# Attention with a fused mixture and MLP on one core: the last head's output is turned and its row sums are made directly in front of a head's first values

## The chip, the cores and the metric

The kernel runs on one core of a Trainium2 chip. The time is the device time of one execution in microseconds (us), and lower is better. Five engines work side by side, each through its own queue in program order, and meet only through semaphores. TensorE (PE) multiplies, VectorE (DVE) and ScalarE (ACT) work on what it leaves in PSUM, GpSimd (POOL) works on tiles in SBUF, and SyncE (SP) issues the transfers.

## The reference, cut to what matters

Three stages follow each other. The change lies in the first; the second and third (a mixture of four causal attention experts, and a two-layer MLP) take its output.

```
batch, n_heads, seq, head_dim = (4, 8, 1152, 64)
q_pool = q.reshape(B, H, S // 2, 2, D).mean(axis=3)         # 576 queries of 1152
scores = scale * np.matmul(q_pool, k.transpose(0, 1, 3, 2)) # 576 x 1152 for each of 32 heads
scores = scores - np.max(scores, axis=-1, keepdims=True)
attn = np.exp(scores)
attn = attn / (np.sum(attn, axis=-1, keepdims=True) + 1e-09)
x = np.matmul(attn, v)
```

Everything is float32. There are 32 heads (4 batches of 8), numbered 0 to 31 here.

## The kernel before

`attention` walks through the 32 heads in a hand-written software pipeline. While head h makes its exponentials, head h + 1 gets its maxima.

The **maxima** (`max_piece`, L329 to L341 on PE, L597 to L601 on DVE) are 15 pieces a head, numbered 0 to 14: PE writes a 128 x 384 block of scores into one of two PSUM banks (L339), and DVE reduces it to one number a row (L600). The two banks alternate. Piece n therefore waits at L338 until DVE has reduced piece n - 2 (`max_freed`), and DVE's reduction of n waits for PE's piece n.

The **scores** of a key tile j (`score(h, j)`, L343 to L361, nine a head) are two matmuls of L349 and two of L358 into one of two double banks. ACT makes the exponentials from them (L529, `exp_done`). `score(h, j)` waits for the exponentials of tile j - 2.

The **values** (`values`, L363 to L376) multiply the exponentials by v into `o_bank`, first for key tiles 0 to 3 (`EARLY` = 4), later for tiles 4 to 8. Each wants a tile's `exp_done`.

After a head, ACT copies the output out of `o_bank` as `oT` (L537, `o_copied`), and DVE adds up the probabilities over the keys (`add_late` and `sum_blocks`, L609 to L628), for which it waits for POOL's additions (`add_tiles`, L239 to L252). The result lies in `group_sums`. One head later PE makes `turn_out` (three fp32 transposes of `oT`, L383) and `sum_rows` (one fp32 matmul of `group_sums`, L388, which the trace counts as two), both into the bank `turn`. When `sum_rows` is done, DVE's `normalise` (L630 to L655) takes the reciprocal and writes the head's rows to `x_all`. DVE has it in its queue between the reductions of pieces 8 and 9 (L679). The next keys may be turned into `turn` only when `normalise` has set `x_ready` (`claim_turn`, L289).

Order on PE is the order of the loop at L403. Before the change `turn_out` stands between pieces 5 and 6, `sum_rows` between pieces 6 and 7, and `score(h, 4)` between 7 and 8; then come `values(h, range(EARLY))` and pieces 9 and 10. Head 0 has no earlier head, so its loop runs without the two.

In head 31 there are no more maxima. In their place stands the beginning of the experts (`first(0, ...)`): `x` 0 to 3 and `x_last` transpose `x_all` (L1225), ACT and DVE split the result (L39, L44). Their banks are two in turn: `x` 3 takes the bank of `x` 1, and `x_last` that of `x` 2, when DVE's split of it is done.

In heads 8 to 14 POOL also splits the experts' weights after its additions (`split_expert`, `split_values`, `split_V`, L274 to L279).

Of the kernel before, what the change touches and what calls it, by code (L numbers as in the profile page):

```python
# [53 lines left out]
def attention(nc, q, k, v, x_all, x_ready, ident, ident_r, ready, ahead):  # L54
# [42 lines left out]
    def max_no(h, n):  # L97
        return h * MAX_USES + n

    ctx = ExitStack()  # L100
    with ctx:
# [186 lines left out]
        def _(pe):  # L288
# [54 lines left out]
            def score(h, j):  # L343
                u, n = h % 2, h * KT + j
                if n >= 2:
                    pe.wait_ge(exp_done, n - 1)
                out = scores[n % 2]
                for half in range(2):
                    nc.tensor.matmul(out[:, half, 0:HALF], kT[u][:, j * P:(j + 1) * P],  # L349
                                     qT[h % 3][:, half * HALF:(half + 1) * HALF],  # L350
                                     start=True, stop=False)
                if j == 0:
                    pe.wait_ge(k1_copied, h + 1)
                    for use in (Q_LO, Q_LO_LAST):
                        at = max_no(h, use)
                        pe.wait_ge(max_freed[at % 2], at // 2 + 1)
                for half in range(2):
                    mm = nc.tensor.matmul(out[:, half, 0:HALF], kT1[u][:, j * P:(j + 1) * P],  # L358
                                          qTm[u][:, half * HALF:(half + 1) * HALF],
                                          start=False, stop=True)  # L360
                mm.then_inc(scores_ready, 1)  # L361

            def values(h, tiles):  # L363
                u = h % 2
                if tiles[0] == 0:
                    pe.wait_ge(v_loaded[u], 16 * (h // 2 + 1))
                    pe.wait_ge(qa_copied, min(h + 3, HEADS))
                for j in tiles:
                    pe.wait_ge(exp_done, h * KT + j + 1)
                    for half in range(2):  # L370
                        at = half * SHIFT
                        mm = nc.tensor.matmul(o_bank[half * D:(half + 1) * D, at:at + HALF],  # L372
                                              v_raw[u][:, j, :],
                                              pT[:, j, half * HALF:(half + 1) * HALF],
                                              start=(j == 0), stop=(j == KT - 1))
                    mm.then_inc(pv_done, 1)  # L376

            def turn_out(h):

                pe.wait_ge(o_copied, h + 1)  # L380
                claim_turn(("out", h))
                for t in range(3):
                    nc.tensor.transpose(turn[:, t * P:(t + 1) * P], oT[:, t * P:(t + 1) * P],  # L383
                                        ident[:, :])

            def sum_rows(h):
                pe.wait_ge(groups_summed, h + 1)
                mm = nc.tensor.matmul(turn[:, 3 * P:3 * P + QT * GROUPS], all_groups[:, :],  # L388
                                      group_sums[:, :], start=True, stop=True)
                mm.then_inc(turned, 1)  # L390
# [12 lines left out]
            for h in range(HEADS - 1):  # L403
                more2 = h + 2 < HEADS

                def maxima(a, z):
                    for at in range(a, z):
                        max_piece(h + 1, at)

                score(h, 0)  # L410
                maxima(0, 2)
                turn_keys(h + 1, "kc", [KT - 1])
                score(h, 1)
                maxima(2, 3)
                score(h, 2)
                maxima(3, 4)
                if more2:
                    turn_queries(h + 2)
                maxima(4, 5)
                score(h, 3)  # L420
                maxima(5, 6)
                if h > 0:
                    turn_out(h - 1)
                maxima(6, 7)
                if h > 0:
                    sum_rows(h - 1)
                maxima(7, 8)
                score(h, 4)
                maxima(8, 9)
                values(h, range(EARLY))  # L430
                maxima(9, 11)
                score(h, 5)
                maxima(11, 12)
                if more2:
                    turn_keys(h + 2, "ka", range(0, 4))
                maxima(12, 13)
                score(h, 6)
                maxima(13, 14)
                score(h, 7)
                maxima(14, 15)  # L440
                score(h, 8)
                if more2:
                    turn_keys(h + 2, "kb", range(4, 8))
                turn_q_lo_m(h + 1)
                values(h, range(EARLY, KT))

            first, h = ahead.tensor(pe, first=True), HEADS - 1
# [4 lines left out]
            first(0, ("x", 1))  # L452
            score(h, 3)
            first(0, ("x", 2))
            turn_out(h - 1)
            sum_rows(h - 1)
            first(0, ("x", 3))
            score(h, 4)
            first(0, ("x_last",))
            values(h, range(EARLY))  # L460
            score(h, 5)
            first(0, ("qk", 0, 0))
# [133 lines left out]
        def _(dve):  # L596
# [33 lines left out]
            def normalise(h):  # L630
                dve.wait_ge(turned, turn_no["out", h] + 1)
                sums = turn[:, 3 * P:3 * P + QT * GROUPS].rearrange("p (t g) -> p t g", g=GROUPS)
                nc.vector.tensor_tensor(picked[:, :, :], sums, own_group[:, :].unsqueeze(1
                                        ).to_broadcast([P, QT, GROUPS]), ALU.mult
                                        ).then_inc(sums_picked, 1)
                dve.wait_ge(sums_picked, 2 * h + 1)
                nc.vector.tensor_reduce(sum_inv[:, :], picked[:, :, :], AX.X, ALU.add
                                        ).then_inc(sums_picked, 1)
                dve.wait_ge(sums_picked, 2 * h + 2)
                nc.vector.reciprocal(sum_inv[:, :], sum_inv[:, :]).then_inc(inverted, 1)  # L640
                dve.wait_ge(inverted, h + 1)
                cols = slice(h * D, (h + 1) * D)
                src = turn[:, 0:3 * P].rearrange("p (t a d) -> p a t d", a=2, d=D)
                by = sum_inv[:, 0:QT - 1].rearrange("p (a t) -> p a t", a=2)
                nc.vector.tensor_tensor(
                    x_all[:, 0:QT - 1, cols].rearrange("p (a t) d -> p a t d", a=2),
                    src[:, :, 0:2, :], by.unsqueeze(3).to_broadcast([P, 2, 2, D]), ALU.mult
                    ).then_inc(x_full, 1)
                nc.vector.tensor_tensor(x_all[0:LAST, QT - 1, cols], src[0:LAST, 1, 2, :],
                                        sum_inv[0:LAST, QT - 1:QT].to_broadcast([LAST, D]),  # L650
                                        ALU.mult)
                dve.wait_ge(x_full, h + 1)
                nc.vector.tensor_tensor(x_all[0:SHIFT, 2, cols], src[0:SHIFT, 0, 2, :],
                                        sum_inv[0:SHIFT, 2:3].to_broadcast([SHIFT, D]),
                                        ALU.mult).then_inc(x_ready, 1)  # L655
# [29 lines left out]
            def add_tile(j, n):  # L685

                total, h = p_sum[:, 0:SQ], HEADS - 1
                dve.wait_ge(exp_done, h * KT + j + 1 if j < KT else HEADS * KT)
                if j == KT:
                    dve.wait_ge(part_summed, h * (len(ON_POOL) - 1) + len(LAST_ON_POOL) - 1)  # L690
                if n == 0:
                    ins = nc.vector.scalar_tensor_tensor(
                        total, pT[:, LAST_ON_POOL.stop, :], EPS / P, pT[:, j, :], ALU.add, ALU.add)
                else:
                    dve.wait_ge(p_summed, h * SUM_STEPS + n)
                    ins = nc.vector.tensor_tensor(total, total, pT[:, j, :], ALU.add)
                ins.then_inc(p_summed, 1)

            first, h = ahead.vector(dve, first=True), HEADS - 1
            first(0, ("x", 0))  # L700
            first(0, ("x", 1))
            first(0, ("x", 2))
            normalise(h - 1)
            first(0, ("x", 3))
            first(0, ("x_last",))
            add_tile(5, 0)
            first(0, ("qk", 0, 0))
            add_tile(6, 1)
# [1121 lines left out]
```

## Time and profile before

| | us |
|---|---|
| median of 3 runs | 1202.93 (1200.16 to 1203.36) |
| the profiled execution, its own time | 1200.94 |
| its span, first to last instruction | 1199.2 |
| PE, DVE, ACT, POOL busy | 1141.5, 650.0, 543.9, 521.9 |
| attention: turning of the first head's output to that of the last | 45.1 to 533.4 |

Times in the trace are microseconds from the start of the span. The ends of matmuls are modelled: a matmul begins before the one ahead of it has ended, so the distance from start to start tells what PE spends on it. A row of the timeline merges instructions of one kind ("x4"); the bracket gives the idle time ahead and what ended it. Where PE waits for a bank, this shows at the weight load (PEld) or at the matmul, as idle time with DVE as its releaser, and often only as a larger distance from start to start.

### The profile page before, as it was taken

The numbers are of one execution on the slowest core, as the hardware profiler recorded it, in microseconds if no ns is written. First come the engines' busy times: TensorE is split into PE (matmuls) and PEld (weight loads), VectorE is DVE, ScalarE is ACT, GpSimd is POOL, SyncE is SP. The second block draws the span as 40 slices with busy tenths as digits, with TensorE's granted clock in tenths as the row PEclk, the third lists the DMA queues.
The fourth block names the chain that finished last, engine by engine and source line by source line (L and its number), as shares of the span: only waits on it lengthen the run. The fifth ranks groups of instructions, "written<-read, shape, count | busy, mean of one in ns | idle before, by whom it ended". The sixth has DMA issues, their size and how long they took to land. (4 is left out here: it accounts for less than half of the span.)

```text
span 1199.2 us, 19574 instructions
## 1 busy us (share of the span) xinstructions
PE 1141.5 (95%) x7232; PEld 956.5 (80%) x7232; DVE 650.0 (54%) x1380; ACT 543.9 (45%) x1131; POOL 521.9 (44%) x560
## 2 busy tenths in 40 slices
PE   6999999989999999998899999789999999999998
PEld 4777777777778777777777777579898989899896
DVE  4788877767888888856556565554121212122120
ACT  4666665565666666546565656633020201111010
POOL 5788899998888888734333333200000000000000
PEclk9999999999999999998999999989999999999999
DMA  8111112211122111003001010132100101010000
GB/s 203 50 54 51 57 60 60 60 43 49 60 60 61 60 60 40 21 1 141 1 1 41 1 41 27 41 123 84 53 1 15 39 1 52 0 52 0 27 1 27
DMA packets 47559, 54.56 MB, mean 46 GB/s; under 512 B 10992, under 2 KB 29424, under 8 KB 46960
## 3 DMA queue, kind: packets, MB, share of 16 engines
q1 hardware_dynamic: 47472, 53.42, 14.3%
q8 instruction: 53, 0.87, 0.3%
q14 instruction: 34, 0.28, 0.1%
HBM read 43.97 MB, written 9.44 MB: 45 GB/s over the span
## 5 line engine op out<-in xcount | busy, mean ns | idle before, releaser
L600 DVE TENSOR_REDUCE part_max<-psA 128x1 f32<-128x384 f32 x480 | 258.4, 556 | 67.9 <-PE psA L339 46.8
L529 ACT ACTIVATE pT<-psA 128x576 f32<-128x576 f32 x288 | 187.7, 652 | 165.5 <-PE psA L358 156.4
L251 POOL TENSOR_TENSOR pT<-pT 128x576 f32<-128x576 f32 x157 | 225.0, 1433 | 25.8 <-ACT pT L529 4.0
L339 PE MATMUL psA<-kT,qT 128*128 128x384 f32 x480 | 174.5, 388 | 11.3 <-DVE part_max L600 10.9
L372 PE MATMUL psA<-pT,v_raw 128*64 128x288 f32 x1152 | 153.9, 412 | 0.0
L1706 ACT ACTIVATE hid_hi<-psC 128x384 fp32r<-128x384 f32 x96 | 47.2, 492 | 198.4 <-PE psC L1631 198.3
L349 PE MATMUL psA<-qT,kT 128*128 128x288 f32 x576 | 133.5, 314 | 0.0
L1725 DVE SCALAR_TENSOR_TENSOR hid_lo<-psC,hid_hi 128x384 fp32r<-128x384 f32 x96 | 53.5, 558 | 137.8 <-ACT hid_hi L1706 137.8
L358 PE MATMUL psA<-qTm,kT 128*128 128x288 f32 x576 | 124.1, 297 | 0.2 <-ACT qTm L515 0.2
L339 PEld LDWEIGHTS psA<-kT,qT 128*128 128x128 f32 x480 | 88.4, 193 | 40.0 <-DVE part_max L600 21.2
L372 PEld LDWEIGHTS psA<-pT,v_raw 128*64 128x64 f32 x1152 | 77.1, 137 | 53.1 <-issue 6.4
L349 PEld LDWEIGHTS psA<-qT,kT 128*128 128x128 f32 x576 | 99.2, 190 | 18.3 <-issue 14.0
L1647 PE MATMUL psC<-w_hi,hid_hi 128*128 128x512 f32 x288 | 113.7, 395 | 0.0
L1647 PE MATMUL psC<-w_hi,hid_lo 128*128 128x512 f32 x288 | 112.5, 391 | 0.0
L1647 PE MATMUL psC<-w_lo,hid_hi 128*128 128x512 f32 x288 | 112.3, 390 | 0.0
L358 PEld LDWEIGHTS psA<-qTm,kT 128*128 128x128 f32 x576 | 93.4, 191 | 0.5 <-issue 0.5
L1631 PE MATMUL psC<-uT_hi,w_hi 128*128 128x384 f32 x384 | 83.1, 339 | 1.4 <-DVE uT_lo L44 1.4
L1631 PE MATMUL psC<-uT_lo,w_hi 128*128 128x384 f32 x384 | 82.9, 338 | 0.0
L1631 PE MATMUL psC<-uT_hi,w_lo 128*128 128x384 f32 x384 | 82.3, 337 | 0.0
L1088 POOL TENSOR_SCALAR moe_probs<-moe_probs,moe_sum_inv,gate 128x128 f32<-128x128 f32 (+4 forms) x80 | 53.3, 666 | 65.3 <-DVE moe_sum_inv L1461 61.2
L1351 ACT ACTIVATE moe_probs<-psB,moe_neg_max 128x128 f32<-128x128 f32 (+4 forms) x80 | 45.5, 569 | 68.0 <-DVE moe_neg_max L1474 67.3
L1631 PEld LDWEIGHTS psC<-uT_hi,w_hi 128*128 128x128 f32 x384 | 68.6, 190 | 2.2 <-DVE uT_lo L44 1.8
(162 smaller groups left out, 1931.7 us busy)
## 6 DMA issues: line engine op xcount, KB each, us to landing
k_raw<-in_k SPq DMA_DIRECT2D x32, 288.0 KB, 2.9
v_raw<-in_v SPq DMA_DIRECT2D x32, 288.0 KB, 2.8
q_raw<-in_q SPq DMA_DIRECT2D x32, 256.0 KB, 3.2
w_raw<-in_moe_w_ch SPq DMA_DIRECT2D x1, 4096.0 KB, 14.0
u_rows<-x_all SPq DMA_DIRECT2D x16, 256.0 KB, 2.0
w_raw<-in_moe_w_ch SPq DMA_DIRECT2D x16, 256.0 KB, 2.7
u_first<-u_rows SPq DMA_DIRECT2D x3, 768.0 KB, 4.5
u_second<-u_rows SPq DMA_DIRECT2D x3, 768.0 KB, 4.8
```

What stands on the lines that cost most here:

```text
L251: nc.gpsimd.tensor_tensor(pT[:, KT, :], pT[:, KT, :], pT[:, j, :], ALU.add).then_inc(part_summed, 1)
L339: nc.tensor.matmul(maxes[n % 2][:, 0:PIECE], qT[h % 3][:, t * P:(t + 1) * P], kT[u][:, c * PIECE:(c + 1) * PIECE], start=True, stop=True). ...
L349: nc.tensor.matmul(out[:, half, 0:HALF], kT[u][:, j * P:(j + 1) * P], qT[h % 3][:, half * HALF:(half + 1) * HALF], start=True, stop=False)
L358: mm = nc.tensor.matmul(out[:, half, 0:HALF], kT1[u][:, j * P:(j + 1) * P], qTm[u][:, half * HALF:(half + 1) * HALF], start=False, stop=True)
L372: mm = nc.tensor.matmul(o_bank[half * D:(half + 1) * D, at:at + HALF], v_raw[u][:, j, :], pT[:, j, half * HALF:(half + 1) * HALF], start=( ...
L529: nc.scalar.activation(pT[:, j, :].rearrange("p (a c) -> p a c", a=2), scores[n % 2][:, :, 0:HALF], ACT.Exp, scale=0.5 * float(D) ** -0.5) ...
L600: nc.vector.tensor_reduce(part_max[u][:, t, c:c + 1], maxes[n % 2][:, 0:PIECE], AX.X, ALU.max).then_inc(max_freed[n % 2], 1)
L1088: nc.gpsimd.tensor_scalar(p, p, sum_inv[0:rows, e, i:i + 1], gate[b % 2][0:rows, i, e:e + 1], ALU.mult, ALU.mult).then_inc(scaled, 1)
L1631: mm = nc.tensor.matmul(up[f % 4], w1_s[w][:, k, f * P:(f + 1) * P], uT[x][:, k, :], start=((w, x, k) == (*PARTS3[0], 0)), stop=((w, x, k) ...
L1647: mm = nc.tensor.matmul(down[t], hid[h][:, f, t * P:(t + 1) * P], w2_s[w][:, f, :], start=(n == 0), stop=(n == 3 * FC - 1))
L1706: nc.scalar.activation(hid[0][:, f, :], up[f % 4], ACT.Relu).then_inc(up_hi, 1)
L1725: nc.vector.scalar_tensor_tensor(hid[1][:, f, :], up[f % 4], 0.0, hid[0][:, f, :].bitcast(F32), ALU.max, ALU.subtract).then_inc(up_lo, 1)
```

## The change

`turn_out(h - 1)` and `sum_rows(h - 1)` move behind piece 8, to stand directly in front of `values(h, range(EARLY))`. `score(h, 4)` moves from behind piece 7 to behind piece 6. In head 31 the two stand behind `x_last` instead of behind `x` 2, and DVE's `normalise` of head 30 moves behind the splits of `x` 3 and `x_last`. No instruction is added or taken away, and DVE's order in the other heads is as it was.

```diff
@@ -418,15 +418,13 @@
                     turn_queries(h + 2)
                 maxima(4, 5)
                 score(h, 3)
-                maxima(5, 6)
+                maxima(5, 7)
+                score(h, 4)
+                maxima(7, 9)
+
                 if h > 0:
                     turn_out(h - 1)
-                maxima(6, 7)
-                if h > 0:
                     sum_rows(h - 1)
-                maxima(7, 8)
-                score(h, 4)
-                maxima(8, 9)
                 values(h, range(EARLY))
                 maxima(9, 11)
                 score(h, 5)
@@ -452,11 +450,11 @@
             first(0, ("x", 1))
             score(h, 3)
             first(0, ("x", 2))
-            turn_out(h - 1)
-            sum_rows(h - 1)
             first(0, ("x", 3))
             score(h, 4)
             first(0, ("x_last",))
+            turn_out(h - 1)
+            sum_rows(h - 1)
             values(h, range(EARLY))
             score(h, 5)
             first(0, ("qk", 0, 0))
@@ -700,9 +698,9 @@
             first(0, ("x", 0))
             first(0, ("x", 1))
             first(0, ("x", 2))
-            normalise(h - 1)
             first(0, ("x", 3))
             first(0, ("x_last",))
+            normalise(h - 1)
             add_tile(5, 0)
             first(0, ("qk", 0, 0))
             add_tile(6, 1)
```

PE's queue in the loop of head 1 before the change, from score 3 to the pieces behind the values. `kT0,qT2` are the operands of the maxima's pieces (of head 2), `qT1,kT1` and `qTm1,kT11` those of the scores (of head 1); L383 is `turn_out`, L388 `sum_rows`, L372 the values:

```order
L349 MATMUL psA<-qT1,kT1 128x288 x2
L358 MATMUL psA<-qTm1,kT11 128x288 x2
L339 MATMUL psA<-kT0,qT2 128x384
L383 MATMUL psA<-ident,oT 128x128 x3
L339 MATMUL psA<-kT0,qT2 128x384
L388 MATMUL psA<-group_sums,all_groups 128x20
L339 MATMUL psA<-kT0,qT2 128x384
L349 MATMUL psA<-qT1,kT1 128x288 x2
L358 MATMUL psA<-qTm1,kT11 128x288 x2
L339 MATMUL psA<-kT0,qT2 128x384
L372 MATMUL psA<-pT,v_raw1 64x288 x8
L339 MATMUL psA<-kT0,qT2 128x384 x2
```

Each of the four pieces 5 to 8 (L339) has other work of PE in front of it. The same place after the change:

```order
L349 MATMUL psA<-qT1,kT1 128x288 x2
L358 MATMUL psA<-qTm1,kT11 128x288 x2
L339 MATMUL psA<-kT0,qT2 128x384 x2
L349 MATMUL psA<-qT1,kT1 128x288 x2
L358 MATMUL psA<-qTm1,kT11 128x288 x2
L339 MATMUL psA<-kT0,qT2 128x384 x2
L383 MATMUL psA<-ident,oT 128x128 x3
L388 MATMUL psA<-group_sums,all_groups 128x20
L372 MATMUL psA<-pT,v_raw1 64x288 x8
L339 MATMUL psA<-kT0,qT2 128x384 x2
```

Pieces 6 and 8 now follow directly on pieces 5 and 7, score 4 alone stands between the two pairs, and L383 and L388 come between piece 8 and the values. This place recurs in heads 1 to 30; head 0 has it without L383 and L388.

PE's queue in head 31 before the change, from score 2 to the first values. L1225 are the transposes `x` 1, 2, 3 and, with 64 columns, `x_last`:

```order
L349 MATMUL psA<-qT1,kT1 128x288 x2
L358 MATMUL psA<-qTm1,kT11 128x288 x2
L1225 MATMUL psB<-ident,x_all 128x128 x4
L349 MATMUL psA<-qT1,kT1 128x288 x2
L358 MATMUL psA<-qTm1,kT11 128x288 x2
L1225 MATMUL psB<-ident,x_all 128x128 x4
L383 MATMUL psA<-ident,oT 128x128 x3
L388 MATMUL psA<-group_sums,all_groups 128x20
L1225 MATMUL psB<-ident,x_all 128x128 x4
L349 MATMUL psA<-qT1,kT1 128x288 x2
L358 MATMUL psA<-qTm1,kT11 128x288 x2
L1225 MATMUL psB<-ident,x_all 128x64 x4
L372 MATMUL psA<-pT,v_raw1 64x288 x8
```

And after the change, where the lines behind the loop have moved up by two (L1223 is L1225 of before):

```order
L349 MATMUL psA<-qT1,kT1 128x288 x2
L358 MATMUL psA<-qTm1,kT11 128x288 x2
L1223 MATMUL psB<-ident,x_all 128x128 x4
L349 MATMUL psA<-qT1,kT1 128x288 x2
L358 MATMUL psA<-qTm1,kT11 128x288 x2
L1223 MATMUL psB<-ident,x_all 128x128 x8
L349 MATMUL psA<-qT1,kT1 128x288 x2
L358 MATMUL psA<-qTm1,kT11 128x288 x2
L1223 MATMUL psB<-ident,x_all 128x64 x4
L383 MATMUL psA<-ident,oT 128x128 x3
L388 MATMUL psA<-group_sums,all_groups 128x20
L372 MATMUL psA<-pT,v_raw1 64x288 x8
```

The eight transposes of `x` 2 and `x` 3 now stand together, and L383 and L388 stand between `x_last` and the values.

## Rows read from the trace of the kernel before

**Rows 1.** The page: busy us of each engine, share of the span, instructions.

```profile
PE 1141.5 (95%) x7232; PEld 956.5 (80%) x7232; DVE 650.0 (54%) x1380; ACT 543.9 (45%) x1131; POOL 521.9 (44%) x560
```

**Rows 2.** One line's instructions, L388 on PE, stretches 168:288 and 287:503.

```profile
L388 PE MATMUL psA<-group_sums,all_groups x16: 181/224/267, 168.4 to 287.7; 128*128 128x20 f32 x16
...
L388 PE MATMUL psA<-group_sums,all_groups x30: 181/224/267, 287.7 to 502.1; 128*128 128x20 f32 x30
```

**Rows 3.** Timeline of PE in head 17: start, us, engine, line, operation.

```profile
302.35 0.34 PE L339 MATMUL psA<-kT,qT 128*128 128x384 f32 x1
302.53 0.49 PE L383 MATMUL psA<-ident,oT 128*128 128x128 f32 x3
...
303.03 0.29 PE L388 MATMUL psA<-group_sums,all_groups 128*128 128x20 f32 x2
303.34 0.44 PE L339 MATMUL psA<-kT,qT 128*128 128x384 f32 x1
...
304.14 0.34 PE L339 MATMUL psA<-kT,qT 128*128 128x384 f32 x1
304.41 2.16 PE L372 MATMUL psA<-pT,v_raw 128*64 128x288 f32 x16
306.50 0.62 PE L339 MATMUL psA<-kT,qT 128*128 128x384 f32 x2
```

**Rows 4.** Timeline of DVE in the same head, three windows.

```profile
302.73 1.06 DVE L600 TENSOR_REDUCE part_max<-psA 128x1 f32<-128x384 f32 x2 [0.15 <-PE psA L339]
...
304.52 0.56 DVE L600 TENSOR_REDUCE part_max<-psA 128x1 f32<-128x384 f32 x1
...
306.98 2.89 DVE L600 TENSOR_REDUCE part_max<-psA 128x1 f32<-128x384 f32 x5 [0.68 <-PE psA L339]
```

**Rows 5.** Timeline of head 0: PE, then PEld and DVE.

```profile
29.81 0.73 PE L339 MATMUL psA<-kT,qT 128*128 128x384 f32 x2
30.80 0.45 PE L339 MATMUL psA<-kT,qT 128*128 128x384 f32 x1 [0.26 <-DVE part_max L600]
31.08 0.43 PE L349 MATMUL psA<-qT,kT 128*128 128x288 f32 x2
...
31.62 0.33 PE L339 MATMUL psA<-kT,qT 128*128 128x384 f32 x1
...
30.09 0.19 PEld L339 LDWEIGHTS psA<-kT,qT 128*128 128x128 f32 x1 [0.23 <-DVE part_max L600]
...
30.19 1.02 DVE L600 TENSOR_REDUCE part_max<-psA 128x1 f32<-128x384 f32 x2
```

**Rows 6.** PE in head 0, the values.

```profile
31.88 2.16 PE L372 MATMUL psA<-pT,v_raw 128*64 128x288 f32 x16
```

**Rows 7.** Timeline of PE in head 31, then a row of DVE there.

```profile
516.70 0.49 PE L383 MATMUL psA<-ident,oT 128*128 128x128 f32 x3
517.03 0.30 PE L388 MATMUL psA<-group_sums,all_groups 128*128 128x20 f32 x2
517.24 0.66 PE L1225 MATMUL psB<-ident,x_all 128*128 128x128 f32 x4
...
518.37 0.45 PE L1225 MATMUL psB<-ident,x_all 64*128 64x64 f32 x4
518.74 2.16 PE L372 MATMUL psA<-pT,v_raw 128*64 128x288 f32 x16
...
516.49 0.69 DVE L44 TENSOR_TENSOR xT_lo<-psB,xT_hi 128x512 fp32r<-128x512 f32 x1 [0.34 <-ACT xT_hi L39]
```

**Rows 8.** PE behind the last `sum_rows`, of head 31.

```profile
535.07 0.30 PE L388 MATMUL psA<-group_sums,all_groups 128*128 128x20 f32 x2
535.21 0.31 PE L1235 MATMUL psB<-wvg_hi,xT_hi 128*64 128x260 f32 x1
```

**Rows 9.** POOL at the end of head 17.

```profile
313.32 1.42 POOL L218 TENSOR_TENSOR k_parts<-k_raw,k_parts 128x576 fp32r<-128x576 f32 x1 [1.61 <-ACT k_parts L483]
```

**Rows 10.** Waits in head 10's stretch, 184.7:201.3.

```profile
DVE p_sum L618 <- POOL pT L251: 1.3, 1, 1.3
```

## The prediction, on record before the changed kernel ran

> **What bounds the kernel now.** I read the page's busy line first: the reader is to see PE at 95% of the span, DVE at 54% and POOL at 44% [rows 1]. So what counts is the distance between starts on PE. Next came the spacing of `sum_rows` over the heads. In the stretch from 287.7 there are 15 of them (30 matmuls) with 214.4 us between the first and the last, 15.31 a head. In the stretch from 168.4 there are eight (16 matmuls) with 119.3 us between them, 17.04 a head, although PE does the same there [rows 2]. These seven periods are set by POOL: in head 10 the additions of `p_sum` on DVE wait 1.3 for POOL [rows 10], where in head 17 POOL itself has 1.61 idle [rows 9]. The others are PE's.
>
> Then the timelines of the place that changes, in heads 17 and 0. I count from the start of piece 5. In head 17 the values start at 304.41 - 302.35 = 2.06 [rows 3]. In head 0, which has neither `turn_out` nor `sum_rows`, they start at 31.88 - 29.81 = 2.07 [rows 5, 6]. This is the row that decides the case: the two operations cost nothing today. In head 0 PE stands idle instead, at piece 6 (0.23 ahead of its weight load) and at piece 7 (0.26 as the view counts it), both released by DVE [rows 5]. In head 17 piece 7 starts at 303.34, which is 0.05 behind the end of reduction 5 (302.73 + 0.56; the row of two, 1.06, ends at 303.79) [rows 3, 4]. So pieces 5 to 7 go at DVE's pace, and the transposes fill holes.
>
> **The change, part by part.** Nothing is added or taken away; the sum consists of holes that open and work that loses its cover. I build up heads 1 to 30 from piece 5, at 0.
>
> Piece 6 now follows at once. It needs reduction 4. Head 0 has this very sequence: 30.09 - 29.81 = 0.28 [rows 5]. Score 4 follows a piece that was just released: 31.08 - 30.80 = 0.28, and takes 31.62 - 31.08 = 0.54 [rows 5]. So piece 7 starts at 0.28 + 0.28 + 0.54 = 1.10. It needs reduction 5, which starts 0.38 behind piece 5 and ends at 0.94 [rows 3, 4]: no wait. That is the gain of the change: score 4 covers the wait at piece 7.
>
> Piece 8 follows at once too, and needs reduction 6. Reductions 5 and 6, back to back, take 1.02 [rows 5], so 6 ends at 0.38 + 1.02 = 1.40, and with the 0.05 of a release piece 8 starts at 1.45. PE could have had it at 1.10 + 0.18 (302.53 - 302.35) [rows 3] = 1.28: a new hole of 0.17, and another 0.10 because the work behind a released piece starts 0.28 and not 0.18 later.
>
> Now `turn_out` and `sum_rows` stand uncovered. `turn_out` starts at 1.45 + 0.28 = 1.73. From it to `sum_rows` PE takes 517.03 - 516.70 = 0.33 [rows 7]: 2.06. From `sum_rows` to the values: the trace has no such pair. The values start about 0.07 ahead of the modelled end of what precedes them, behind a piece (304.14 + 0.34 against 304.41) [rows 3] as behind `x_last` (518.37 + 0.45 against 518.74) [rows 7]. `sum_rows` lasts 0.29 or 0.30 [rows 3, 7], so I take 0.22. The values then start at 2.28, against 2.06: **0.22 us later a head**. From below: 0.14 to the next matmul, as behind the last `sum_rows` [rows 8], and 0.18 in place of 0.28 behind piece 8, which gives 2.10, or +0.04. From above: 0.31 behind `sum_rows`, as it is to piece 7 (303.34 - 303.03), and 1.06 for the two reductions [rows 3, 4], which gives 2.41, or +0.35.
>
> On the values' start the Trainium skill (TensorE: Matmul & The Clock Gate, Part 2, step 5, NX overlap) says that the drain of a matmul overlaps the fill of the next. By that the values should follow `sum_rows` at the 0.14 of the lower bound, and a head would lose 0.14. The trace disagrees at the values: both times they wait for nearly all of the modelled end. Step 1 of the same part of the Trainium skill's page says that PE pulls weight loads ahead of matmuls in flight; for a released piece the trace does not show it, since in head 0 the load of piece 6 begins at 30.09, on release. By that rule the 0.28 would be 0.18 and a head would lose 0.12.
>
> Is it given back later? DVE is not late: reduction 8 ends near 2.5 (it began at 2.17 before [rows 3, 4] and begins some 0.2 earlier), `turned` comes at 2.06 + 0.29 = 2.35, so `normalise` has no new wait, although it now depends on a matmul that stands directly ahead of it. After it DVE had 0.68 idle until reduction 9, which waits for piece 9 on PE [rows 4]; that only grows. Pieces 9 and 10 stand behind the values (306.50), and everything to the end of the head hangs on them. Score 4 is ready earlier, and so are its exponentials on ACT, but nobody waits for these. The keys' turning needs `x_ready`, which comes a little earlier. The exponentials behind score 5 come 0.22 later for POOL, which at the end of the head has 1.61 to spare [rows 9]. So PE keeps the 0.22.
>
> Where it counts: 30 heads have the new place, 7 of their periods are POOL's and swallow it (they lose 12 us to POOL, 119.3 - 7 x 15.31, much more than 7 x 0.22). 23 x 0.22 = **+5.1**.
>
> Head 0 has nothing to uncover: its piece 8 starts at 1.45, is released, so it lasts 0.44 to 0.45 (30.80's row) [rows 5], and the values follow 0.07 ahead of the end: 1.82 against 2.07, **-0.25**.
>
> Head 31: `turn_out` and `sum_rows` stood where `x` 3 would have waited for DVE anyway: it starts at 517.24, 0.06 behind DVE's split of `x` 1 (516.49 + 0.69) [rows 7]. That hole stays. The two now come between `x_last` and the values: 0.33 + 0.22, less about 0.09, since `turn_out` can start closer behind a transpose than the values do. **+0.46**, between 0.33 and 0.64. `normalise` behind two splits of DVE is hidden: the next addition waits for exponentials.
>
> The sum: 5.1 - 0.25 + 0.46 = +5.3. The profiled execution took 1200.94 (its span 1199.2 and 1.7 around it), so 1206.2. The median of the runs is 1202.93, 0.17% above it. On that scale the forecast is 1202.93 + 5.3 = **1208.2 us**. The bounds a head give 23 x 0.04 + 0.1 = +1.0 and 23 x 0.35 + 0.4 = +8.4: 1203.9 to 1211.3.
>
> **The rivals.**
> A dearer one: all 30 heads pay, because the delay comes behind the additions that POOL's chain needs. 30 x 0.22 + 0.2 = +6.8, 1209.7. Against it: POOL works through without waiting in these heads.
> A cheaper one: the released weight load or the change to the values costs less than I take. At 0.04 to 0.14 a head it is +1.1 to +3.4, say 1205.2, inside what a measurement can tell (0.3%, 3.6 us). For it: [rows 8]. Against it: both starts of the values.
> One on the other side, faster: PE's sum of work decides and not the pace of DVE. From `turn_out` to piece 7 the old order takes 303.34 - 302.53 = 0.81 [rows 3]; without piece 6 (0.18) that leaves 0.63 for two fp32 groups with fp32r matmuls on either side. Together in front of the fp32 values they take 0.33 + 0.14 = 0.47. That would save 0.16 in each of 23 heads, -3.7, so 1199.2. It decides if reductions 5 and 6 come early enough that piece 8 needs no wait, by 1.28 where I count 1.40. Against it: head 0's 2.07 without either group shows that the 0.63 was no cost.
> That the change does not do what it says can be left aside; the order of the queue shows it.
>
> **How the numbers follow.** My forecast 0.66, the dearer rival 0.12, the cheaper one 0.17, the faster one 0.05. Slower 0.78, same 0.17, faster 0.05. The range takes in both bounds of a head and a run's scatter (1200.16 to 1203.36 before): 1203.5 to 1211.5, which leaves out the faster rival and the tails.
>
> **What would show it.** In a middle head, from piece 5: piece 6 at 0.28, piece 7 near 1.10, piece 8 near 1.45 with DVE named as releaser, the values near 2.28; 15.53 a head in place of 15.31, and an unchanged 17.0 in the seven heads of POOL. Head 0's values at 1.82. Wrong would be: values at 2.06 or earlier (the sum of work decides), or 0.22 at the values and yet 15.31 a head (given back later, at DVE or POOL).

## The result and the profile after

The median went from 1200.96 to 1207.44 us in 15 runs of each. The ratio is 1.0047, with a 95% interval of 1.0035 to 1.0060: the change costs 4 to 7 us, about 5.6 (the two medians lie 6.5 apart). The forecast was +5.3. The profiled execution took 1209.26, its span is 1207.5. The granted clock of TensorE is 1.00, the upper of its two levels (2.4 GHz), up to the end of attention in the trace of before and in that of after, so it has no part in what attention loses.

The place that changed, in head 17 of the kernel after, is the counterpart of [rows 3] (start, us, engine, line, operation; L339 pieces, L349 the first two matmuls of score 4, L383 `turn_out`, L388 `sum_rows`, L372 values):

```profile
305.04 0.72 PE L339 MATMUL psA<-kT,qT 128*128 128x384 f32 x2
305.59 0.42 PE L349 MATMUL psA<-qT,kT 128*128 128x288 f32 x2
...
306.12 0.87 PE L339 MATMUL psA<-kT,qT 128*128 128x384 f32 x2
306.83 0.49 PE L383 MATMUL psA<-ident,oT 128*128 128x128 f32 x3
307.16 0.30 PE L388 MATMUL psA<-group_sums,all_groups 128*128 128x20 f32 x2
307.38 2.16 PE L372 MATMUL psA<-pT,v_raw 128*64 128x288 f32 x16
```

The values start 2.34 behind piece 5, where they started at 2.06. Next come the weight loads of the two pieces that follow directly on another (PEld), and DVE's reductions 5 and 6, 7 and 8, and the first step of `normalise`, counterparts of [rows 4]:

```profile
305.31 0.19 PEld L339 LDWEIGHTS psA<-kT,qT 128*128 128x128 f32 x1 [0.22 <-DVE part_max L598]
...
306.54 0.19 PEld L339 LDWEIGHTS psA<-kT,qT 128*128 128x128 f32 x1 [0.34 <-issue]
...
305.41 1.02 DVE L598 TENSOR_REDUCE part_max<-psA 128x1 f32<-128x384 f32 x2
...
306.50 1.09 DVE L598 TENSOR_REDUCE part_max<-psA 128x1 f32<-128x384 f32 x2
307.50 0.17 DVE L631 TENSOR_TENSOR picked<-psA,own_group 128x20 f32<-128x20 f32 x1
```

Piece 6 waits for reduction 4 (0.22 idle). Piece 8 waits for reduction 6, which ends at 305.41 + 1.02 = 306.43; its load begins at 306.54, with 0.34 idle ahead of it. The view puts that hole down to "issue" and names no engine. What ends in it is a wait that stands as an instruction of its own, of line 338 (`max_freed`), and that runs right behind the end of reduction 6:

```profile
L338 PEldq EVENT_SEMAPHORE  x1: 51/51/51, 306.5 to 306.5; - x1
```

`sum_rows` as it recurs, against [rows 2], for the heads of POOL and for those behind them:

```profile
L388 PE MATMUL psA<-group_sums,all_groups x16: 185/226/266, 173.1 to 291.6; 128*128 128x20 f32 x16
...
L388 PE MATMUL psA<-group_sums,all_groups x30: 185/226/266, 291.6 to 509.8; 128*128 128x20 f32 x30
```

Fourteen periods of 218.2 are 15.59 a head in place of 15.31. The seven periods of POOL take 118.5 in place of 119.3: they swallow the delay, although in most of these heads too the values start 2.35 behind piece 5. Head 31, the counterpart of [rows 7]:

```profile
522.77 0.66 PE L1223 MATMUL psB<-ident,x_all 128*128 128x128 f32 x4
523.81 0.66 PE L1223 MATMUL psB<-ident,x_all 128*128 128x128 f32 x4 [0.38 <-DVE xT_lo L44]
...
524.93 0.45 PE L1223 MATMUL psB<-ident,x_all 64*128 64x64 f32 x4
525.31 0.55 PE L383 MATMUL psA<-ident,oT 128*128 128x128 f32 x3
525.69 0.30 PE L388 MATMUL psA<-group_sums,all_groups 128*128 128x20 f32 x2
525.92 2.16 PE L372 MATMUL psA<-pT,v_raw 128*64 128x288 f32 x16
```

`x` 3 still starts 1.04 behind `x` 2, now with an open wait in between; before it was 517.24 [rows 7] - 516.20:

```profile
516.20 0.66 PE L1225 MATMUL psB<-ident,x_all 128*128 128x128 f32 x4
```

From `x_last` to the values it takes 0.99, where it took 0.37: +0.62.

The span grew by 8.3, more than the ratio of the runs. Of this, 1.2 is there before the changed place is reached for the first time (piece 5 of head 0's loop starts at 31.02 in place of 29.81), and 1.1 lies behind attention. Neither stands in the change, and both vary as much between kernels that do not differ there: over the twelve traces of this case piece 5 of head 0's loop starts between 28.4 and 31.2, and from head 31's first values to the end it takes 677 to 683 (680.5 before, 681.6 after), in the old order and the new one alike. The changed places themselves make up -0.2 (head 0), 22 x 0.275 = 6.1 (the periods of heads 1 to 8 and 16 to 29), and 0.9 from head 30 to the experts; the seven heads of POOL came out 0.8 shorter.

### The profile page after: what moved, and what is told of

Its sections match the earlier page's. It is cut to its first block and busy times, and to the rows that moved or that the text cites. A ratio compares the mean times of both kernels' runs of the same rounds, so it can differ in the third digit from the quotient of the medians.

```text
span 1207.5 us, 19574 instructions
## 1 busy us (share of the span) xinstructions
PE 1146.6 (95%) x7232; PEld 956.3 (79%) x7232; DVE 645.7 (53%) x1380; ACT 543.9 (45%) x1131; POOL 521.4 (43%) x560
## 5 line engine op out<-in xcount | busy, mean ns | idle before, releaser
L339 PE MATMUL psA<-kT,qT 128*128 128x384 f32 x480 | 172.4, 387 | 12.1 <-DVE part_max L598 8.7
L372 PE MATMUL psA<-pT,v_raw 128*64 128x288 f32 x1152 | 153.8, 412 | 0.0
L349 PE MATMUL psA<-qT,kT 128*128 128x288 f32 x576 | 133.4, 313 | 0.0
L339 PEld LDWEIGHTS psA<-kT,qT 128*128 128x128 f32 x480 | 88.2, 193 | 50.5 <-issue 25.4
L372 PEld LDWEIGHTS psA<-pT,v_raw 128*64 128x64 f32 x1152 | 77.0, 136 | 47.8 <-issue 0.2
L349 PEld LDWEIGHTS psA<-qT,kT 128*128 128x128 f32 x576 | 99.2, 190 | 18.3 <-issue 14.0
```

The source lines that it names most:

```text
L339: nc.tensor.matmul(maxes[n % 2][:, 0:PIECE], qT[h % 3][:, t * P:(t + 1) * P], kT[u][:, c * PIECE:(c + 1) * PIECE], start=True, stop=True). ...
```

## The experiments

Theory: **cover**. Without other work between the pieces PE waits for DVE at pieces 6 and 7, as head 0 of before shows. In the old order `turn_out` and `sum_rows` fill the wait at piece 6 and most of that at piece 7; the new order takes the fillers out, puts score 4 ahead of piece 7, and leaves waits open at pieces 6 and 8. Rivals: the **sum of work** on PE decides; or the **new neighbours** cost the 0.28 (fp32 transposes ahead of the values). Positions are read in head 17 from the start of piece 5, unless said otherwise. In heads 1 to 8 and 17 to 29 of a trace the start of the values agrees within 0.03, but for one head of one trace; "a head" is the mean period behind POOL's heads.

The first seven kernels were executed once each: 1207.85, 1212.93, 1210.05 and 1207.97 us for the two with added transposes, score 4 back, and the second wait moved, next to 1203.32 of before, then 1188.64, 1191.72 and 1204.28 (short reductions in the old and the new order, head 31 alone), next to a median of 1200.77 of before. One such time scatters by several us, more than most of these edits are worth, so the positions decide.

### Work added in the place of the transposes

```diff
-                for t in range(3):
+                for t in (0, 1, 2, 0, 1, 2):
                     nc.tensor.transpose(turn[:, t * P:(t + 1) * P], oT[:, t * P:(t + 1) * P],
```

In the old order: 

> The order of before, with turn_out's three transposes made twice (six transposes, the same result). One look, read in a middle head from the start of piece 5. Theory (cover: in the old order the transposes fill a wait of PE for DVE): the three extra transposes are 0.33 of PE's work, but about 0.15 to 0.2 of it fits into what is left of the wait ahead of piece 7, so the values start at 2.16 to 2.25 in place of 2.07, and a head lasts 15.4 to 15.5. Rival (sum of work: PE's own work decides, no cover): the full 0.33, values at 2.40, a head 15.65.

In the new order: 

> The order of after, with turn_out's three transposes made twice. Theory (cover: behind piece 8 nothing waits for DVE any more): the full 0.33 us, values at 2.68 in place of 2.35 behind the start of piece 5, 15.92 a head in place of 15.59. Rival (the 0.28 that the change costs is the price of new neighbours, and a wait is still there that takes up work): less than 0.33, values below 2.60.

The old order, with six transposes:

```profile
304.64 0.34 PE L339 MATMUL psA<-kT,qT 128*128 128x384 f32 x1
304.82 0.82 PE L383 MATMUL psA<-ident,oT 128*128 128x128 f32 x6
305.39 0.42 PE L339 MATMUL psA<-kT,qT 128*128 128x384 f32 x1
305.65 0.29 PE L388 MATMUL psA<-group_sums,all_groups 128*128 128x20 f32 x2
305.79 0.42 PE L339 MATMUL psA<-kT,qT 128*128 128x384 f32 x1
...
306.89 2.16 PE L372 MATMUL psA<-pT,v_raw 128*64 128x288 f32 x16
```

Values at 2.25, 15.50 a head: 0.33 of added work costs 0.19, the rest goes into what was left of the wait. Piece 7 now starts 0.14 behind `sum_rows` (305.79 - 305.65), where it stood 0.31 behind it in [rows 3]: 0.17 of wait was left there, and it is filled. The new order, with six:

```profile
308.42 0.72 PE L339 MATMUL psA<-kT,qT 128*128 128x384 f32 x2
...
311.09 0.46 PE L372 MATMUL psA<-pT,v_raw 128*64 128x288 f32 x2
```

Values at 2.67, 15.92 a head: the full 0.33. This is what the theory says, and it speaks against a wait being left behind piece 8.

### Score 4 back between pieces 7 and 8

```diff
-                maxima(5, 7)
+                maxima(5, 8)
                 score(h, 4)
-                maxima(7, 9)
+                maxima(8, 9)
```

> The order of after, with score 4 back between pieces 7 and 8 (pieces 5, 6, 7, score 4, piece 8, turn_out, sum_rows, values). It undoes the one part that is meant to help. Theory (cover): pieces as in head 0 of before, 6 at 0.29, 7 at 0.99, 8 at 1.81; turn_out 1.99, sum_rows 2.32, values 2.55, which is 0.48 later than before and 0.20 later than after; 15.79 a head. Rival (the place of score 4 does not matter, the price is only at the values): values at 2.35 as in after.

```profile
304.84 0.72 PE L339 MATMUL psA<-kT,qT 128*128 128x384 f32 x2
305.82 0.44 PE L339 MATMUL psA<-kT,qT 128*128 128x384 f32 x1 [0.26 <-DVE part_max L598]
...
306.63 0.34 PE L339 MATMUL psA<-kT,qT 128*128 128x384 f32 x1
306.81 0.49 PE L383 MATMUL psA<-ident,oT 128*128 128x128 f32 x3
307.13 0.30 PE L388 MATMUL psA<-group_sums,all_groups 128*128 128x20 f32 x2
307.36 2.16 PE L372 MATMUL psA<-pT,v_raw 128*64 128x288 f32 x16
```

The pieces stand as in head 0 of before [rows 5], with the same 0.26 for DVE, and the two operations come on top: values at 2.52, 15.76 a head. So moving them alone costs 0.46 a head, and the new place of score 4 gives back 0.17. The rival falls.

### DVE made faster

```diff
-                nc.vector.tensor_reduce(part_max[u][:, t, c:c + 1], maxes[n % 2][:, 0:PIECE],
+                nc.vector.tensor_reduce(part_max[u][:, t, c:c + 1], maxes[n % 2][:, 0:PIECE // 2],
```

In the old order: 

> The order of before, with DVE's reduction of each piece over 192 of its 384 columns (leaves half of the columns out of the maxima); PE's work is as before. A reduction should last about 0.36 in place of 0.56. Theory (cover: PE waits for DVE at piece 7): the wait goes, values at about 1.80 to 1.90 in place of 2.07 behind the start of piece 5. Rival (sum of work decides in the old order): 2.07 stays.

In the new order: 

> The order of after, with DVE's reduction of each piece over 192 of its 384 columns (leaves half of the columns out of the maxima). Theory (cover): without waits for DVE there is nothing to cover, so both orders cost the same work: values at 1.75 to 1.85, within 0.1 of the old order with the same short reductions, and a head as long or up to 0.15 shorter. Rival (the new neighbours cost the 0.28 by themselves): values 0.2 to 0.3 later than in the old order with short reductions.

Old order, then new order, from piece 5 to the values:

```profile
298.19 0.34 PE L339 MATMUL psA<-kT,qT 128*128 128x384 f32 x1
...
300.07 2.16 PE L372 MATMUL psA<-pT,v_raw 128*64 128x288 f32 x16
```

```profile
297.21 0.52 PE L339 MATMUL psA<-kT,qT 128*128 128x384 f32 x2
297.56 0.42 PE L349 MATMUL psA<-qT,kT 128*128 128x288 f32 x2
...
298.10 0.67 PE L339 MATMUL psA<-kT,qT 128*128 128x384 f32 x2
298.60 0.49 PE L383 MATMUL psA<-ident,oT 128*128 128x128 f32 x3
...
299.15 2.16 PE L372 MATMUL psA<-pT,v_raw 128*64 128x288 f32 x16
...
297.58 0.62 DVE L598 TENSOR_REDUCE part_max<-psA 128x1 f32<-128x192 f32 x2 [0.35 <-PE psA L339]
```

With reductions of 0.36 in place of 0.56 the old order has its values at 1.88 (2.06 before) and the new one at 1.94 (2.34). The difference falls from 0.28 to 0.06, and the heads stand at 14.81 and 14.87. The old order lies within what was expected (1.80 to 1.90). The new one misses its range (1.75 to 1.85) by 0.09, and its head is 0.06 longer than the old one's, not as long or shorter: reduction 6 ends only at 298.20, and `turn_out` starts 0.50 behind piece 7 (298.60 - 298.10), where two steps of 0.18 without a wait would make 0.36. So piece 8 still waits a little. Four fifths of the cost depend on DVE's pace; neither the sum of work nor the neighbours explain these. How the last 0.06 divides between that wait and the neighbours no run shows.

### The second wait of piece 8

Piece 8, `(QT - 1, 0)`, is the first to read the last query tile, which is turned and copied together with the last key tile ("kc"). So it has two waits: for DVE, and for that copy, which was made long ago.

```diff
-                for first, name in (((0, 0), "ka"), ((0, 1), "kb"), ((QT - 1, 0), "kc")):
+                for first, name in (((0, 0), "ka"), ((0, 1), "kb"), ((1, 1), "kc")):
```

> The order of after; the wait for the copied last key tile (turn_freed, line 336, long satisfied) stands ahead of piece 5 in place of piece 8, so piece 8 has one wait in place of two. In after piece 8 starts 1.54 behind piece 5, 0.09 later than the 1.45 that was forecast. Theory: the second wait makes the release cost about 0.06 more, since one of the two is an instruction of its own; piece 8 at 1.45 to 1.48 and the values at 2.28 to 2.32, 15.53 a head. Rival: the 0.09 has nothing to do with the number of waits; 1.54 and 2.35 stay.

```profile
304.17 0.73 PE L339 MATMUL psA<-kT,qT 128*128 128x384 f32 x2
...
305.26 0.81 PE L339 MATMUL psA<-kT,qT 128*128 128x384 f32 x2
305.90 0.49 PE L383 MATMUL psA<-ident,oT 128*128 128x128 f32 x3
...
306.46 2.16 PE L372 MATMUL psA<-pT,v_raw 128*64 128x288 f32 x16
...
305.62 0.19 PEld L339 LDWEIGHTS psA<-kT,qT 128*128 128x128 f32 x1 [0.28 <-DVE part_max L598]
```

Piece 8's load begins at 1.45, the values at 2.29, and 15.52 a head: the 0.06 that the forecast was short of, to 0.01. The hole is now put down to DVE, and no wait of line 338 stands in it as an instruction of its own. The page of the profile shows the same for all pieces together. First the group of the weight loads after the change, then with this edit:

```profile
L339 PEld LDWEIGHTS psA<-kT,qT 128*128 128x128 f32 x480 | 88.2, 193 | 50.5 <-issue 25.4
```

```profile
L339 PEld LDWEIGHTS psA<-kT,qT 128*128 128x128 f32 x480 | 88.2, 193 | 49.5 <-DVE part_max L598 34.8
```

### Head 31 alone

The kernel has the loop of before and the two other hunks of the change.

> Only the change in head 31 (turn_out, sum_rows and normalise behind x_last); the loop over the heads is that of before. Theory: 15.31 a head and values at 2.07 as before; in head 31 the values start 6.44 behind the first score, as in after, in place of 5.83: +0.6 us in all, too small for a single time. Rival (head 31's change hides behind DVE): 5.83 stays.

15.32 a head, values at 2.07. In head 31 the first score starts at 513.83 and the values at 520.27, 6.44 later; before they started at 518.74 - 512.91 = 5.83. The +0.6 of the trace comes from this part.

### A better order

```diff
                 maxima(5, 6)
                 if h > 0:
                     turn_out(h - 1)
                 maxima(6, 7)
+                score(h, 4)
+                maxima(7, 8)
                 if h > 0:
                     sum_rows(h - 1)
-                maxima(7, 8)
-                score(h, 4)
                 maxima(8, 9)
                 values(h, range(EARLY))
```

> A version that may beat both: piece 5, turn_out, piece 6, score 4, piece 7, sum_rows, piece 8, values; head 31 as before. Each of the two pairs gets a filler, and score 4 covers the wait at piece 7. Theory (cover): piece 6 at 0.42, score 4 at 0.68, piece 7 at 1.21, sum_rows at 1.47, piece 8 at 1.65, values at 1.92: 0.15 earlier than before, 23 heads of 0.15 make 3.4 us, 0.28% faster than before. Rival (the two kinds of matmuls cost at every change between them, and the old order has as many): values at 2.07 or later, no gain.

```profile
301.53 0.34 PE L339 MATMUL psA<-kT,qT 128*128 128x384 f32 x1
301.71 0.49 PE L383 MATMUL psA<-ident,oT 128*128 128x128 f32 x3
301.96 0.42 PE L339 MATMUL psA<-kT,qT 128*128 128x384 f32 x1
302.21 0.42 PE L349 MATMUL psA<-qT,kT 128*128 128x288 f32 x2
...
302.75 0.34 PE L339 MATMUL psA<-kT,qT 128*128 128x384 f32 x1
302.92 0.29 PE L388 MATMUL psA<-group_sums,all_groups 128*128 128x20 f32 x2
303.12 0.41 PE L339 MATMUL psA<-kT,qT 128*128 128x384 f32 x1
303.46 2.16 PE L372 MATMUL psA<-pT,v_raw 128*64 128x288 f32 x16
```

Every pair of pieces has work between them. Values at 1.93, 15.19 a head, 1197.40 us (median of 12): ratio to before 0.9976 (0.9966 to 0.9987), a gain of 0.24% where 0.28% was expected.

The same idea at piece 11, the other place where a piece waits for DVE. The edit is shown against the mixed order and cut: `turn_half`, which makes two of the four transposes of `turn_keys`, is left out.

```diff
-                maxima(11, 12)
                 if more2:
-                    turn_keys(h + 2, "ka", range(0, 4))
+                    turn_half(h + 2, 0)
+                maxima(11, 12)
+                if more2:
+                    turn_half(h + 2, 1)
                 maxima(12, 13)
```

> The mixed order (piece 5, turn_out, piece 6, score 4, piece 7, sum_rows, piece 8, values), and in the other place where a piece waits for DVE the filler is put into the wait: of the four transposes of the next keys (line 298, behind piece 11 so far) two stand ahead of piece 11 and two behind it. In the mixed order piece 11 starts at 5.11 and piece 12 at 5.69 behind piece 5, although PE is done with score 5 at 5.00. Theory (cover): piece 11 at about 5.17 without a wait, piece 12 at 5.58 to 5.60 (its own wait, for reduction 10, is then the limit), 0.1 less a head, 15.09 in place of 15.19; 2 us less than the mixed order, about 0.45% faster than before. Rival (the wait at piece 11 is so short that a change of operands costs as much): 15.19 stays.

Piece 11 starts at 5.13 and piece 12 at 5.58, 15.11 a head, 1197.79 us (median of 12, ratio 0.9977, 0.9965 to 0.9989). The trace shows the 0.08; the times do not, and the 0.45% that was expected against before came out as 0.23%. The last kernel adds the edit of the second wait to this one:

> As x9_mixed_keys_split, and the long satisfied wait for the copied last key tile stands ahead of piece 5 in place of piece 8. In the mixed order reduction 6 ends at 1.44 and piece 8 starts at 1.58. Theory (two waits release later than one): piece 8 at 1.50 to 1.55, so 0.03 to 0.08 less a head than x9, at most 1.5 us, which only the trace can tell. Rival (in the mixed order piece 8 waits for PE's own work and not for DVE): 1.58 stays.

Piece 8 at 1.52, values at 1.88, 15.06 a head, 1195.72 us (median of 6): ratio 0.9956 (0.9941 to 0.9971). This version, the mixed order with both additions, beats both kernels.

## Why the prediction was right

Direction and mechanism held, and the size nearly so, step by step:

| behind piece 5, or a head | forecast | after |
|---|---|---|
| piece 6 | 0.28 | 0.28 |
| piece 7 | 1.10 | 1.08 |
| piece 8, its load | 1.45 | 1.51 |
| `turn_out`, `sum_rows` | 1.73, 2.06 | 1.79, 2.12 |
| values | 2.28 | 2.34 |
| head 0, values | 1.82 | 1.88 |
| a head of PE | 15.53 | 15.59 |
| head 31 | +0.46 | +0.6 |

**The term that was too small** is piece 8: I took 0.05 for a release (from the end of DVE's reduction to the start of the load that waited for it), as [rows 3, 4] show it at piece 7. Piece 8 has a second wait, and its release costs 0.11; the edit that moves this wait gives the forecast's positions. The 0.22 from `sum_rows` to the values, of which the trace had no case, came out as 0.22. By the Trainium skill (TensorE: Matmul & The Clock Gate, Part 2, step 5, NX overlap) the next matmul fills while the last one drains. That alone does not tell the 0.22: it is there at every start of the values behind `sum_rows`, against 0.14 where a piece follows without a wait (305.79 - 305.65 with six transposes in the old order) and where a matmul of the experts does [rows 8]. The weights of the latter have 64 columns, as those of the values have, so their width is not the reason. The values stand behind waits of their own (`v_loaded`, `qa_copied`, `exp_done`), as piece 8 does, and no run takes them away; why they start later stays open.

**A reading that was too wide**: that pieces 5 to 7 go at DVE's pace today. In head 17 of before only piece 7 is released by DVE. Reductions 3 and 4 end at 301.47 + 1.10 = 302.57, and the load of piece 6 begins only at 302.75, behind the transposes:

```profile
301.47 1.10 DVE L600 TENSOR_REDUCE part_max<-psA 128x1 f32<-128x384 f32 x2
...
302.75 0.19 PEld L339 LDWEIGHTS psA<-kT,qT 128*128 128x128 f32 x1
```

It is head 0 that waits at piece 6. The sum did not use this reading.

**Where it counts** held too: the heads of POOL pay nothing (118.5 for seven periods; 118.2 even in the order that costs 0.46 elsewhere), and the other heads give nothing back later.

**What was luck**: the changed places outside POOL's heads cost 6.8 in the trace (6.1 - 0.2 + 0.9) and not 5.3; 23 times the 0.06 of piece 8 make 1.4 of the difference, head 31 most of the rest. POOL's heads, forecast at no change, came out 0.8 shorter, which brought the sum back to 6.0; over the twelve traces they take 118.2 to 120.8. And 1208.2 was built on a median of 1202.93 from three runs. On the 1200.96 of fifteen the same +5.3 gives 1206.3, against 1207.44, and the dearer rival 1207.8: the times cannot tell these two apart, the periods of POOL's heads do.

**What the view would show** was wrong in one point: the hole ahead of piece 8 does not name DVE but "issue".

**Head 31** was forecast at 0.46. The transition I took as 0.09 shorter is not: `turn_out` starts 0.38 behind `x_last`, whose transposes have 64 rows, and `sum_rows` another 0.38 behind it.

The rivals: the faster one falls with the short reductions, where the new order is still not ahead, and with piece 7's start when work is added; the cheaper and the dearer ones by the positions and the periods above. The interval of the ratio, 4.2 to 7.2 us, holds the 6.0 of the changed places; it would hold 7.1 as well, but the 1.1 behind attention lies within what that stretch varies by.

## What to carry to other kernels

Work that an in-order engine does while it would have waited anyway is free, and moving it to a "tidier" place makes it cost its full time. Before moving it, look for an iteration that runs without it (here head 0): if its marks stand at the same distance, the work is cover. With two alternating banks put something between every two fills, and split the fillers rather than bundle them.

## What the runs showed of the hardware

- The weight load of a piece that waits for DVE begins 0.05 behind the end of the reduction when it has one wait (303.34 before, 305.62 with the second wait moved), and 0.11 behind it when it has two, as piece 8 has (306.54 - 306.43). Then one of the two waits is an instruction of its own in the trace (51 ns), and the view names no releaser.
- Behind a piece that was released the next matmul starts 0.26 to 0.28 later, behind piece 5 of the old order, which had not waited, 0.18. The release alone is not the reason: behind piece 6 of the old order, which did not wait for DVE but follows on the transposes, it is 0.26 too (303.03 - 302.77).
- Behind `sum_rows`, a matmul of 20 columns, the next matmul starts 0.14 later where nothing waits, but the values 0.22 later. The values start 0.07 to 0.08 ahead of the modelled end of what precedes them, behind a piece, `x_last` or `sum_rows`.
- Two reductions that find their data ready take 1.02 together and 0.56 each: DVE starts the second before the first has ended.
